# All visits in the small groups make the states' part of y on four tiles of TensorE, and VectorE adds the two parts; the first units' orders arranged anew

## The chip, the core and the metric

The kernel runs on one core of one Trainium2 chip. The metric is the device time of one execution in microseconds (us), the median of several runs. The profiled execution is one further run under the hardware profiler.

## The reference

A gated linear attention over (batch 4, 8 heads, 768 steps, head size 48) feeds two MLPs over 3072 tokens of width 384.

```
f = 1 / (1 + exp(-f_logit))
for t in range(S):
    state = f[t][:, None] * state + outer(k[t], v[t])
    y[t]  = q[t] @ state
x  = y.transpose(0, 2, 1, 3).reshape(B * S, H * D)          # 3072 x 384
x2 = ((1 / (1 + exp(-(x @ w_gate)))) * (x @ w_val)) @ w_out # d_ff 1536
h  = x2 @ w_in                                              # d_ff 2048
out = (h * (1 / (1 + exp(-1.702 * h)))) @ w_out2
```

## The kernel before

**Attention in units.** A unit is a pair of heads over 256 steps; there are 48 of them. Its 256 steps fall into four chunks of 64. For each unit ScalarE makes the gates (`forget`), VectorE their running product and its reciprocal (`prepare`: a scan and a reciprocal), GpSimd multiplies q by the one and k by the other (`decay_q`, `decay_k`), ScalarE scales q by the product at the end of the chunk before (`prepare_q`, into `q_in`) and takes the chunk ends out (`take_end`).

**Visits.** TensorE works on the units in visits, each for up to three units at different stages: unit n is turned (k transposed, `turn_ps`, and the scores k by q), unit n-1 has its products k by v (from which VectorE makes the states, `new_states`, four in a row), and unit n-2 has its y made: masked scores times v, and the states times `q_in`. The products stand in the two banks of `att_ps` (in the first visits also of `out_ps`). After a visit VectorE masks the scores and makes the states; ScalarE copies y to `y_t` (`take_y`); DMAs move it to `x_raw`, the input of the first MLP. There are 53 visits, v = 0 to 52; the first eight stand before the MLP.

**The MLPs.** All products are made of three fp32r products (high by high, low by high, high by low), so every operand is split: ScalarE casts the high part, VectorE subtracts to get the low part (`x_lo`, `act_lo`, `w_lo`). The tokens go in groups: two small ones of 256, then groups of 512. A group of the first MLP has 12 blocks (`j`); a block has 18 products up (gate and value, into `up_ps`), perhaps a visit, and then the 9 products out of the block before. For each block ScalarE makes the sigmoid (`act_f`), VectorE multiplies (`act_f`), ScalarE casts `act_hi`, VectorE subtracts `act_lo`. Groups 0 and 1 are the small ones: visits 8 to 12 stand in blocks 1, 2, 4, 6, 8 of group 0, visits 13 to 20 in blocks 0, 1, 3, 4, 5, 7, 8, 9 of group 1. In group 0 the weights of the first MLP are loaded and split, too: ScalarE casts `w_hi`, VectorE makes `w_lo`. The first piece of weights is split by GpSimd in thirds (`split_w1`).

**Order.** Each engine's instructions are written out by hand, and each engine runs them in order; semaphores connect the engines.

**Two ways to make y.** Up to visit 20 (`v < APART`) the states' products are added in PSUM to the same columns as the scores' part: TensorE waits until its own earlier products are drained (`tiles_done`), then adds 6 or 8 products, and ScalarE copies y once, 128 x 256. In visits 8 to 20 VectorE waits for that copy before it reads the banks (`copied_first`); elsewhere ScalarE waits until VectorE has read scores and products (`wait_products_read`). From visit 21 on the states' part goes to columns of its own (`STATE_COL`), on four tiles of TensorE without the drain; ScalarE copies that part in four copies of 48 x 128, and VectorE then adds the scores' part out of PSUM (`add_y`). SyncE's move of y and TensorE's next visit wait for `y_copied` in the one form and for `y_added` in the other (`wait_y`).

## Time and profile before

| | |
|---|---|
| median of 3 runs | 951.71 us (951.61 to 951.87) |
| profiled execution | 953.08 us, its span 951.0 us |
| TensorE matmul, busy | 934.9 us (98% of the span) |
| VectorE, busy | 487.0 us (51%) |
| ScalarE, busy | 375.3 us (39%) |
| GpSimd, busy | 105.8 us (11%) |
| chain that ended last | TensorE 95%, VectorE 2%, the rest below 2% each |

The span is the time from the first to the last instruction, and about 2 us of the execution lie around it. TensorE's share is that of the whole; in the first 31 us, where the first units are prepared, it is lower. A time in a timeline is counted from the start of the span. The first product of the MLP starts at 30.75 us; the third group's first visit starts at 141.7 us.

### The profile page before, as it was taken

Reading aid. Unit: us, or ns where it says so; the run is one execution under the profiler, and the core shown is the slowest. Engines: PE = TensorE matmul, PEld = TensorE weight load, DVE = VectorE, ACT = ScalarE, POOL = GpSimd, SP = SyncE. Lnnn points to the kernel's source line nnn. Section 1 sums busy time; section 2 is a strip of 40 time slices with the busy share of each in tenths; the row PEclk is TensorE's granted clock in tenths of the full one; section 3 lists DMA queues with packets and bytes.
Section 4 is the critical chain, followed back from the end, with each engine's and each line's share of the span. In section 5 each row is a group of like instructions: output and inputs, shape, how many; then the busy total and the mean of one; then the engine's idle time right before and its main releaser. Section 6 shows DMA issues by size and latency. Waiting matters only on the chain.

```text
span 951.0 us, 18139 instructions
## 1 busy us (share of the span) xinstructions
PE 934.9 (98%) x7203; PEld 781.2 (82%) x7203; DVE 487.0 (51%) x829; ACT 375.3 (39%) x941; POOL 105.8 (11%) x125
## 2 busy tenths in 40 slices
PE   7899999999999999999999999999999999999997
PEld 5899988888888888888888888888888888888885
DVE  7897776647665665664333234343443443433433
ACT  4665444543444444443424333233232333232332
POOL 4211211101110111110004420000000000000000
PEclk9899999999999999999999999999999999999999
DMA  5762322211112212120123320020010200100000
GB/s 146 201 188 60 85 64 61 64 47 58 57 48 54 80 52 51 29 80 21 63 69 98 99 84 1 1 67 1 24 43 1 68 1 1 66 1 1 34 1 35
DMA packets 44008, 52.36 MB, mean 55 GB/s; under 512 B 8464, under 2 KB 33808, under 8 KB 43920
## 3 DMA queue, kind: packets, MB, share of 16 engines
q1 hardware_dynamic: 41184, 43.30, 15.8%
q10 hardware_dynamic: 2736, 7.85, 2.9%
q8 instruction: 59, 0.97, 0.4%
q14 instruction: 29, 0.24, 0.1%
HBM read 36.96 MB, written 9.44 MB: 49 GB/s over the span
## 4 chain that ended last, share of the span: by engine, by line
PE 95%; DVE 2%; issue 1%; ACT 1%; DMA 1%; SPq 0%; ACTq 0%; POOL 0%; DVEq 0%; POOLq 0%
PE up_ps L1087 17%; PE up_ps L1088 17%; PE up_ps L1089 17%; PE out_ps L1087 13%; PE out_ps L1088 12%; PE out_ps L1089 12%; PE att_ps L1035 2%; PE att_ps L1057 1%; PE att_ps L1047 1%; PE turn_ps L1014 1%; PE up_ps L1003 1%; PE att_ps L1069 1%; PE att_ps L1080 1%; DMA x_raw<-y_t 1%; DVE inv_prod L811 1%
## 5 line engine op out<-in xcount | busy, mean ns | idle before, releaser
L1087 PE MATMUL up_ps<-x_hi,w_hi 128*128 128x512 f32 (+1 forms) x792 | 293.7, 371 | 1.5 <-DVE x_lo L867 0.8
L1089 PE MATMUL up_ps<-x_hi,w_lo 128*128 128x512 f32 (+1 forms) x792 | 293.2, 370 | 0.0
L1088 PE MATMUL up_ps<-x_lo,w_hi 128*128 128x512 f32 (+1 forms) x792 | 293.1, 370 | 0.0
L1087 PE MATMUL out_ps<-act_hi,w_hi 128*128 128x512 f32 (+1 forms) x540 | 208.0, 385 | 0.8 <-DVE act_lo L932 0.8
L1088 PE MATMUL out_ps<-act_lo,w_hi 128*128 128x512 f32 (+1 forms) x540 | 203.2, 376 | 0.0
L1089 PE MATMUL out_ps<-act_hi,w_lo 128*128 128x512 f32 (+1 forms) x540 | 202.9, 376 | 0.0
L718 ACT CAST act_hi<-act_f 128x512 fp32r<-128x512 f32 (+1 forms) x180 | 106.6, 592 | 232.1 <-DVE act_f L923 159.7
L932 DVE TENSOR_TENSOR act_lo<-act_f,act_hi 128x512 fp32r<-128x512 f32 (+1 forms) x180 | 118.1, 656 | 113.8 <-ACT act_hi L718 113.8
L1087 PEld LDWEIGHTS up_ps<-x_hi,w_hi 128*128 128x128 f32 x792 | 149.7, 189 | 27.8 <-DVE x_lo L867 1.3
L1089 PEld LDWEIGHTS up_ps<-x_hi,w_lo 128*128 128x128 f32 x792 | 149.6, 189 | 25.3
L1088 PEld LDWEIGHTS up_ps<-x_lo,w_hi 128*128 128x128 f32 x792 | 149.7, 189 | 25.0
L926 DVE TENSOR_TENSOR act_f<-act_f,up_ps 128x512 f32<-128x512 f32 x96 | 66.0, 688 | 173.3 <-ACT act_f L714 173.3
L714 ACT ACTIVATE act_f<-up_ps 128x512 f32<-128x512 f32 x96 | 57.4, 598 | 192.9 <-PE up_ps L1089 192.9
L1087 PEld LDWEIGHTS out_ps<-act_hi,w_hi 128*128 128x128 f32 x540 | 101.8, 188 | 22.2 <-DVE act_lo L932 1.2
L1089 PEld LDWEIGHTS out_ps<-act_hi,w_lo 128*128 128x128 f32 x540 | 102.0, 189 | 18.6
L1088 PEld LDWEIGHTS out_ps<-act_lo,w_hi 128*128 128x128 f32 x540 | 102.0, 189 | 16.9
L923 DVE TENSOR_TENSOR act_f<-act_f,up_ps 128x512 f32<-128x512 f32 (+1 forms) x84 | 50.3, 599 | 112.5 <-PE up_ps L1089 103.9
L811 DVE RECIPROCAL inv_prod<-prod 128x256 f32<-128x256 f32 x48 | 84.1, 1752 | 1.6
L712 ACT ACTIVATE act_f<-up_ps 128x512 f32<-128x512 f32 (+1 forms) x84 | 45.1, 537 | 62.7 <-PE up_ps L1089 60.7
L506 POOL TENSOR_TENSOR q_dec<-q_raw,prod 128x256 f32<-128x256 f32 x48 | 35.3, 735 | 299.6 <-DVE prod L804 229.9
L639 ACT COPY y_t<-att_ps 48x128 f32<-48x128 f32 x128 | 33.3, 260 | 60.3 <-DVE state L840 59.2
L624 ACT ACTIVATE q_in<-q_dec,p_end 128x64 f32<-128x64 f32 x176 | 47.4, 339 | 0.9
(77 smaller groups left out, 577.7 us busy)
## 6 DMA issues: line engine op xcount, KB each, us to landing
stage<-w SPq DMA_DIRECT2D x16, 384.0 KB, 3.3
stage<-w ACTq DMA_DIRECT2D x9, 576.0 KB, 4.3
q_raw<-q_t SPq DMA_DIRECT2D x96, 48.0 KB, 1.9
k_raw<-k_t SPq DMA_DIRECT2D x96, 48.0 KB, 1.9
v_raw<-v_n SPq DMA_DIRECT2D x48, 96.0 KB, 2.2
x_raw<-x_dram SPq DMA_DIRECT2D x6, 768.0 KB, 5.0
out_t<-final SPq DMA_DIRECT2D x18, 256.0 KB, 2.1
f_raw<-f_t SPq DMA_DIRECT2D x82, 48.0 KB, 1.9
```

What stands on the lines that cost most here:

```text
L506: pool.tensor_tensor(q_dec[:, n % 4, :], q_raw[:, u.s, :], prod[:, u.s, :], ALU.mult).then_inc(q_dec_done, 1)
L624: last = act.mul(q_in[:, n % 2, at], q_dec[:, n % 4, at], end_before(u, c))
L712: act.activation(act_f[:, b.t, 0:b.n], up_ps[:, 0, 0:b.n], ACT.Sigmoid).then_inc(sig_done, 1)
L714: act.activation(act_f[:, b.t, 0:b.n], up_ps[:, b.j % 2, 0:b.n], ACT.Sigmoid, scale=1.702).then_inc(sig_done, 1)
L718: act.copy(act_hi[:, b.t, 0:b.n], act_f[:, b.t, 0:b.n]).then_inc(act_hi_done, 1)
L811: dve.reciprocal(inv_prod[:, u.s, :], prod[:, u.s, :]).then_inc(inv_done, 1)
L923: dve.tensor_tensor(act_f[:, b.t, 0:b.n], act_f[:, b.t, 0:b.n], up_ps[:, 1, 0:b.n], ALU.mult).then_inc(mul_done, 1)
L926: dve.tensor_tensor(act_f[:, b.t, 0:b.n], act_f[:, b.t, 0:b.n], up_ps[:, b.j % 2, 0:b.n], ALU.mult).then_inc(mul_done, 1)
L932: dve.tensor_tensor(act_lo[:, b.t, 0:b.n], act_f[:, b.t, 0:b.n], act_hi[:, b.t, 0:b.n].bitcast(F32), ALU.subtract).then_inc(act_split, 1)
L1087: pe.matmul(dst, w_hi[:, at:at + P], m_hi, start=first, stop=False)
L1088: pe.matmul(dst, w_hi[:, at:at + P], m_lo, start=False, stop=False)
L1089: return pe.matmul(dst, w_lo[:, at:at + P], m_hi, start=False, stop=last)
```

## The change

It has four parts.

1. Every visit from the eighth on (that is, all visits in the small groups too) makes the states' part of y in columns of its own; ScalarE copies that part in four copies and VectorE adds the scores' part. Only the visits before the MLP keep the old form. This concerns visits 9 to 20, twelve in number (visit 8 makes no y). Where the unit is the first of its sequence, two products with a state of zeros are added.
2. In all visits ScalarE copies first, as soon as the visit is done, and VectorE waits for the copy before it reads the banks.
3. On ScalarE and VectorE the first units' steps are in another order: `forget` of units 2 to 5 and the loads of f and w1 come earlier, `prepare(2)` comes ahead of the first visit's mask.
4. On GpSimd a third of the first weights is split before `decay_k(3)`, and two waits for the states are gone.

```diff
-
-    APART = VISIT_AT[2, 0]
...
-        def wait_products_read(eng, v):
-
-            turned, kept, _ = VISITS[v]
-            if turned is not None:
-                eng.wait_ge(scores_masked, turned + 1)
-            if kept is not None:
-                eng.wait_ge(state_done, CH * (kept + 1))
-
-        def copied_first(v):
-
-            return BEFORE_MLP <= v < APART
-
         def wait_y(eng, n):
 
-            if out_visit[n] < APART:
+            if out_visit[n] < BEFORE_MLP:
                 eng.wait_ge(y_copied, n + 1)
             else:
-                eng.wait_ge(y_added, len([m for m in range(n + 1) if out_visit[m] >= APART]))
+                eng.wait_ge(y_added, n - UG + 1)
...
-                    pool.wait_ge(w1_hi_done, 1)
+                    if part == 0:
+                        pool.wait_ge(w1_hi_done, 1)
                     pool.tensor_tensor(w_lo[:, at], w1_staged(0)[:, at], w_hi[:, at].bitcast(F32),
                                        ALU.subtract).then_inc(w1_thirds, 1)
 
...
                 decay(0)
                 decay(1)
                 decay(2)
-                decay(3)
-
-                pool.wait_ge(state_done, CH * 2)
+                decay_q(3)
                 split_w1(0)
+                decay_k(3)
                 split_w1(1)
                 decay_q(4)
-                pool.wait_ge(state_done, CH * 4)
                 split_w1(2)
                 decay_k(4)
                 decay(5)
...
                 def take_y(n):
                     v = out_visit[n]
                     act.wait_ge(visit_done, v + 1)
-                    if not copied_first(v):
-                        wait_products_read(act, v)
                     wait(act, y_moved[n % YS], 16 * moves(n % YS, n))
                     y = y_t[:, n % YS, :].rearrange("p (c r t) -> p c r t", c=BLOCKS, r=SIDES)
-                    if v < APART:
+                    if v < BEFORE_MLP:
                         act.copy(y, banks(v)[:, :, Y_COL:STATE_COL].rearrange("p r (c t) -> p c r t", c=BLOCKS)).then_inc(y_copied, 1)
                         return
                     for i in range(PAIR):
...
                 first_load_f(2)
                 forget(1)
                 first_load_f(3)
+                forget(2)
                 take_end(0)
                 take_k(0)
-                forget(2)
+                forget(3)
                 first_load_f(4)
+                load_w1(0)
+                prepare_q(0)
                 take_end(1)
-                prepare_q(0)
                 take_k(1)
-                forget(3)
-                load_w1(0)
+                first_load_f(5)
+                take_end(2)
+                forget(4)
                 prepare_q(1)
-                take_end(2)
                 take_k(2)
-                first_load_f(5)
+                load_w1(1)
                 w1_first_part(0)
                 take_y(0)
                 take_end(3)
+                prepare_q(2)
                 take_k(3)
-                load_w1(1)
-                prepare_q(2)
-                forget(4)
+                forget(5)
                 take_y(1)
                 prepare_q(3)
                 first_load_f(6)
                 load_w1(2)
-                forget(5)
                 take_y(2)
                 first_move_y(2, slice(2, None))
                 take_y(3)
...
                 def add_y(n, v):
 
 
-                    dve.wait_ge(y_copied, n + 1)
                     y = y_t[:, n % YS, :].rearrange("p (c r t) -> p r c t", c=BLOCKS, r=SIDES)
                     dve.tensor_tensor(y, y, banks(v)[:, :, Y_COL:STATE_COL].rearrange("p r (c t) -> p r c t", c=BLOCKS),
                                       ALU.add).then_inc(y_added, 1)
...
                 def after_visit(v):
                     turned, kept, made = VISITS[v]
                     dve.wait_ge(visit_done, v + 1)
-                    if made is not None and copied_first(v):
-                        wait_y(dve, made)
+                    if made is not None:
+                        dve.wait_ge(y_copied, made + 1)
                     if turned is not None:
                         mask(turned, v)
                     if kept is not None:
                         new_states(kept, v)
-                    if made is not None and v >= APART:
+                    if made is not None and v >= BEFORE_MLP:
                         add_y(made, v)
...
                 dve.wait_ge(gaps_set, 8)
                 prepare(0)
                 prepare(1)
+                prepare(2)
                 after_visit(0)
-                prepare(2)
                 after_visit(1)
                 prepare(3)
                 after_visit(2)
...
-                    if made is not None and v < APART:
+                    if made is not None and v < BEFORE_MLP:
 
                         last.then_inc(tiles_done, 1)
                         pe.wait_ge(tiles_done, made + 1)
```

A visit on TensorE in block 4 of the first small group, before (`scores` times `v_raw` and `q_in` by `state` make y):

```order
L1035 MATMUL att_ps<-scores,v_raw 48x64 [waits y_copied,scores_masked,state_done]
L1035 MATMUL att_ps<-scores,v_raw 48x64 x7
L1047 MATMUL att_ps<-v_raw,k_rows 64x48 [waits v_loaded2,k_rows_done]
L1047 MATMUL att_ps<-v_raw,k_rows 64x48 x7
L1057 MATMUL att_ps<-q_dec,k_dec 64x64 [waits q_dec_done]
L1057 MATMUL att_ps<-q_dec,k_dec 64x64 x7
L1069 MATMUL att_ps<-q_in,state 48x64 [waits q_in_done,state_done,tiles_done]
L1069 MATMUL att_ps<-q_in,state 48x64 x7
```

The same visit after the change:

```order
L1017 MATMUL att_ps<-scores,v_raw 48x64 [waits y_added,scores_masked,state_done]
L1017 MATMUL att_ps<-scores,v_raw 48x64 x7
L1029 MATMUL att_ps<-v_raw,k_rows 64x48 [waits v_loaded2,k_rows_done]
L1029 MATMUL att_ps<-v_raw,k_rows 64x48 x7
L1039 MATMUL att_ps<-q_dec,k_dec 64x64 [waits q_dec_done]
L1039 MATMUL att_ps<-q_dec,k_dec 64x64 x7
L1062 MATMUL att_ps<-q_in,state 48x64 [waits q_in_done,state_done]
L1062 MATMUL att_ps<-q_in,state 48x64 x7
```

The wait for `tiles_done` is gone, and the wait at the visit's first product into `att_ps` is for `y_added`, not for `y_copied`.

ScalarE around the same visit, from `act_hi` of block 4 to the next sigmoid, before:

```order
L718 CAST act_hi<-act_f 128x256 [waits act_used,mul_done]
L607 COPY k_rows<-turn_ps 128x256 [waits k_turned]
L612 COPY p_end<-prod 128x4 [waits scan_done]
L635 COPY y_t<-att_ps 128x256 [waits y_moved2,visit_done]
L624 ACTIVATE q_in<-q_dec,p_end 128x64 [waits p_end_done,visit_done,q_dec_done]
L624 ACTIVATE q_in<-q_dec,p_end 128x64 x3
L588 ACTIVATE gate<-f_raw 128x4x63 [waits scan_done,f_loaded0]
L589 ACTIVATE floor<-f_raw 128x4
L569 CAST w_hi<-final 128x1152 [waits w1_loaded3]
L563 DMA stage<-w 128x1152 [waits w1_split]
```

And after:

```order
L701 CAST act_hi<-act_f 128x256 [waits act_used,mul_done]
L592 COPY k_rows<-turn_ps 128x256 [waits k_turned]
L597 COPY p_end<-prod 128x4 [waits scan_done]
L622 COPY y_t<-att_ps 48x2x64 [waits y_moved2,visit_done]
L622 COPY y_t<-att_ps 48x2x64 x3
L609 ACTIVATE q_in<-q_dec,p_end 128x64 [waits p_end_done,visit_done,q_dec_done]
L609 ACTIVATE q_in<-q_dec,p_end 128x64 x3
L573 ACTIVATE gate<-f_raw 128x4x63 [waits scan_done,f_loaded0]
L574 ACTIVATE floor<-f_raw 128x4
L554 CAST w_hi<-final 128x1152 [waits w1_loaded3]
L548 DMA stage<-w 128x1152 [waits w1_split]
```

One copy of y has become four, and they stand in the same place, ahead of `q_in`, the gates of a later unit, a weight's high part and the sigmoid (`act_f`).

VectorE behind the mask of that visit, before:

```order
L822 TENSOR_TENSOR scores<-att_ps,causal 128x256 [waits y_copied,visit_done]
L840 SCALAR_TENSOR_TENSOR state<-state,p_end,att_ps 128x48 [waits p_end_done]
L840 SCALAR_TENSOR_TENSOR state<-state,p_end,att_ps 128x48 [waits state_done] x3
L923 TENSOR_TENSOR act_f<-act_f,up_ps 128x256 [waits value_ready,sig_done]
L874 TENSOR_TENSOR w_lo<-final,w_hi 128x1152 [waits w1_hi_done]
L932 TENSOR_TENSOR act_lo<-act_f,act_hi 128x256 [waits act_hi_done]
```

And after:

```order
L805 TENSOR_TENSOR scores<-att_ps,causal 128x256 [waits y_copied,visit_done]
L823 SCALAR_TENSOR_TENSOR state<-state,p_end,att_ps 128x48 [waits p_end_done]
L823 SCALAR_TENSOR_TENSOR state<-state,p_end,att_ps 128x48 [waits state_done] x3
L830 TENSOR_TENSOR y_t<-y_t,att_ps 128x2x2x64
L905 TENSOR_TENSOR act_f<-act_f,up_ps 128x256 [waits value_ready,sig_done]
L856 TENSOR_TENSOR w_lo<-final,w_hi 128x1152 [waits w1_hi_done]
L914 TENSOR_TENSOR act_lo<-act_f,act_hi 128x256 [waits act_hi_done]
```

The add of y stands behind the states and ahead of the next block's `act_f`.

GpSimd in the front, from `q_dec` of unit 3 to `k_dec` of unit 4, before:

```order
L506 TENSOR_TENSOR q_dec<-q_raw,prod 128x256 [waits scan_done,q_loaded1]
L514 TENSOR_TENSOR k_dec<-k_raw,inv_prod 128x256 [waits visit_done,inv_done,k_loaded1]
L526 TENSOR_TENSOR w_lo<-stage,w_hi 128x384 [waits w1_hi_done,state_done]
L526 TENSOR_TENSOR w_lo<-stage,w_hi 128x384 [waits w1_hi_done]
L506 TENSOR_TENSOR q_dec<-q_raw,prod 128x256 [waits visit_done,scan_done,q_loaded0]
L526 TENSOR_TENSOR w_lo<-stage,w_hi 128x384 [waits w1_hi_done,state_done]
L514 TENSOR_TENSOR k_dec<-k_raw,inv_prod 128x256 [waits visit_done,inv_done,k_loaded0]
```

And after:

```order
L492 TENSOR_TENSOR q_dec<-q_raw,prod 128x256 [waits scan_done,q_loaded1]
L513 TENSOR_TENSOR w_lo<-stage,w_hi 128x384 [waits w1_hi_done]
L500 TENSOR_TENSOR k_dec<-k_raw,inv_prod 128x256 [waits visit_done,inv_done,k_loaded1]
L513 TENSOR_TENSOR w_lo<-stage,w_hi 128x384
L492 TENSOR_TENSOR q_dec<-q_raw,prod 128x256 [waits visit_done,scan_done,q_loaded0]
L513 TENSOR_TENSOR w_lo<-stage,w_hi 128x384
L500 TENSOR_TENSOR k_dec<-k_raw,inv_prod 128x256 [waits visit_done,inv_done,k_loaded0]
```

The first third of `w_lo` has moved ahead of `k_dec` of unit 3, and no third waits for `state_done` any more.

## Rows read from the trace of the kernel before

**Rows 1.** Busy time by stretch: us, then each engine, granted clock, DMA share, GB/s.

```profile
31.00:80.00 49.00, 45.95 (x593) 43.75 (x593) 45.75 (x72) 30.16 (x85) 9.05 (x13) 0.97 0.57 163
80.00:141.00 61.00, 60.00 (x874) 55.78 (x873) 43.10 (x92) 28.85 (x102) 11.38 (x16) 1.00 0.27 72
141.00:450.00 309.00, 309.00 (x3150) 254.09 (x3149) 189.70 (x341) 138.97 (x434) 43.15 (x58) 1.00 0.20 54
```

**Rows 2.** Timeline of TensorE, a small group's visit (start us, length us, what).

```profile
53.48 0.43 PE L1057 MATMUL att_ps<-q_dec,k_dec 48*64 48x64 f32 x16
...
54.58 0.39 PE L1087 MATMUL out_ps<-act_hi,w_hi 128*128 128x256 f32 x1
```

**Rows 3.** Timeline of TensorE, a large group's visit.

```profile
142.47 0.43 PE L1057 MATMUL att_ps<-q_dec,k_dec 48*64 48x64 f32 x16
...
143.05 0.39 PE L1087 MATMUL out_ps<-act_hi,w_hi 128*128 128x256 f32 x1
```

**Rows 4.** Timeline of ScalarE, blocks 6 and 7 of the first small group.

```profile
62.93 0.41 ACT L718 CAST act_hi<-act_f 128x256 fp32r<-128x256 f32 x1 [2.27 <-DVE act_f L923]
...
63.61 0.38 ACT L635 COPY y_t<-att_ps 128x256 f32<-128x256 f32 x1
...
66.28 0.39 ACT L712 ACTIVATE act_f<-up_ps 128x256 f32<-128x256 f32 x1
```

**Rows 5.** Timeline of VectorE, first small group (in brackets: idle before, releaser).

```profile
49.72 0.42 DVE L923 TENSOR_TENSOR act_f<-act_f,up_ps 128x256 f32<-128x256 f32 x1 [0.55 <-PE up_ps L1089]
...
62.54 0.36 DVE L923 TENSOR_TENSOR act_f<-act_f,up_ps 128x256 f32<-128x256 f32 x1
...
64.95 0.41 DVE L822 TENSOR_TENSOR scores<-att_ps,causal 128x256 f32<-128x256 f32 x1
...
66.70 0.42 DVE L923 TENSOR_TENSOR act_f<-act_f,up_ps 128x256 f32<-128x256 f32 x1 [0.26 <-ACT act_f L712]
```

**Rows 6.** Timeline of ScalarE, the four copies of y in a large group.

```profile
145.77 1.08 ACT L639 COPY y_t<-att_ps 48x128 f32<-48x128 f32 x4 [1.92 <-DVE state L840]
```

**Rows 7.** Timeline of VectorE, the add in a large group.

```profile
146.88 0.42 DVE L848 TENSOR_TENSOR y_t<-y_t,att_ps 128x256 f32<-128x256 f32 x1 [1.27 <-ACT y_t L639]
```

**Rows 8.** Waits of VectorE, 80 to 140 us: us in total, times, longest.

```profile
DVE scores L822 <- ACT y_t L635: 3.8, 8, 0.9
```

**Rows 9.** Timeline of VectorE, second small group.

```profile
93.39 0.42 DVE L822 TENSOR_TENSOR scores<-att_ps,causal 128x256 f32<-128x256 f32 x1 [0.29 <-ACT y_t L635]
...
95.30 0.42 DVE L923 TENSOR_TENSOR act_f<-act_f,up_ps 128x256 f32<-128x256 f32 x1 [0.41 <-PE up_ps L1089]
...
114.10 0.42 DVE L923 TENSOR_TENSOR act_f<-act_f,up_ps 128x256 f32<-128x256 f32 x1 [1.28 <-PE up_ps L1089]
...
127.57 0.42 DVE L923 TENSOR_TENSOR act_f<-act_f,up_ps 128x256 f32<-128x256 f32 x1 [1.40 <-PE up_ps L1089]
...
132.68 0.42 DVE L923 TENSOR_TENSOR act_f<-act_f,up_ps 128x256 f32<-128x256 f32 x1 [1.52 <-PE up_ps L1089]
```

**Rows 10.** Timeline of SyncE's DMA issues, the last visit before the third group.

```profile
131.92 1.16 SPq L401 DMA_DIRECT2D x_raw<-y_t  x2
```

**Rows 11.** Timeline of VectorE, front.

```profile
20.21 0.69 DVE L804 TENSOR_TENSOR_SCAN prod<-gate,floor 128x256 f32<-128x256 f32 x1 [2.00 <-ACT floor L589]
```

**Rows 12.** Timeline of ScalarE, front.

```profile
16.18 1.15 ACT L569 CAST w_hi<-stage 128x1152 fp32r<-128x1152 f32 x1 [1.19 <-DMA stage<-w]
```

**Rows 13.** Timeline of GpSimd, front.

```profile
17.05 0.72 POOL L514 TENSOR_TENSOR k_dec<-k_raw,inv_prod 128x256 f32<-128x256 f32 x1 [1.05 <-issue]
18.28 1.96 POOL L526 TENSOR_TENSOR w_lo<-stage,w_hi 128x384 fp32r<-128x384 f32 x2 [0.51 <-DVE state L840]
```

**Rows 14.** Chain that ended last, front: start us, length us, what.

```profile
26.52 4.93 DMA x_raw<-y_t
```

**Rows 15.** Timeline of TensorE, the first visit that makes y in a small group.

```profile
43.06 0.44 PE L1035 MATMUL att_ps<-scores,v_raw 64*48 64x64 f32 x16 [1.49 <-issue]
```

**Rows 16.** Busy time by stretch, behind that visit.

```profile
44.00:49.00 5.00, 4.95 (x40) 4.88 (x41) 4.89 (x9) 3.34 (x11) 1.15 (x2) 0.66 0.26 45
```

## The prediction

> **What bounds the kernel now.** I read the share of each engine by stage first, then the timelines of the engines that wait on each other there. From 141 us on TensorE is busy for all of the time [rows 1], so nothing that the edit does to the large groups' visits can come out there, unless it makes TensorE wait. What can move the end lies before 141 us: the front, up to the first MLP product at about 31 us, and the two small groups (256 tokens; blocks of 27 products), 31 to 141 us. There VectorE is nearly as full as TensorE: 45.75 against 45.95 us of the 49 us up to 80 us, 43.10 against 60.00 us in the 61 us behind them [rows 1]. The first small group (weights are split in it too) is thus bound by two things at once, the second mostly by TensorE with stretches that VectorE holds up.
>
> **The visits on TensorE.** In a small group's visit the next out product starts 1.10 us behind the start of the scores' products (53.48 to 54.58) [rows 2]; in a visit of the large groups, whose form the small ones now take, 0.58 us behind it (142.47 to 143.05) [rows 3]. The drain wait and the two-bank form go: 0.52 us for each of the 12 visits (v = 9 to 20), 6.2 us in all. For the three units of a batch's first step two more matmuls of 64 columns are added, some hundredths each. This is a gain only where TensorE is what the others wait for.
>
> **What the same visits cost ScalarE and VectorE.** ScalarE's one copy of y (0.38 us) [rows 4] becomes four, which take 1.08 us in the large groups [rows 6]: 0.70 us more. VectorE adds the states' part afterwards: 0.42 us, of which some 0.34 us are its own when the next operation starts overlapped [rows 7].
>
> In the first small group ScalarE works without a gap from act_hi at 62.93 over the copy of y at 63.61 to the next sigmoid at 66.28 [rows 4], and VectorE's next act_f waits 0.26 us for that sigmoid [rows 5]. So ScalarE's 0.70 us are on the path from act_f at 62.54 to act_f at 66.70. VectorE's add is hidden: it fits in the 0.26 us and the 0.70 us of new idle. Its mask at 64.95 isn't delayed, as the four copies would end at 63.61 + 1.08 = 64.69. Behind it VectorE is back to back, so nothing is given back, and TensorE, 0.52 us quicker, waits for the sigmoid. Three visits are like this (blocks 4, 6, 8): 2.1 us. At block 2 VectorE waited 0.55 us for TensorE before 49.72 [rows 5], part of which covers the longer chain: I count 0.4 of the 0.7 us. The first visit makes no y. The sum for the first small group is +2.5 us. It is at least +2.0 (TensorE, relieved, catches up some of it at the end of the group) and at most +3.3 us, if an operation behind the copies doesn't overlap with them and each visit costs 0.1 us more, and block 2 the whole.
>
> In the second small group VectorE waits for the copy of y at all eight visits, 3.8 us in total [rows 8]. Where the copy stands right behind ScalarE's other work, that wait is 0.29 us, as at 93.39 [rows 9], and the four copies move the mask by some 0.66 us. Where the wait is longer (3.8 - 8 x 0.29 = 1.5 us in all), the copy had waited for the visit's end, which now comes 0.52 us sooner, and that much is covered. So the masks come 8 x 0.66 - 1.5 = 3.8 us later and the adds bring 8 x 0.34 = 2.7 us: 6.5 us on VectorE's chain. Four of the visits have idle behind them in which VectorE waited for TensorE, 0.41, 1.28, 1.40 and 1.52 us [rows 9], and the earlier TensorE lets the chain use it up: 0.4 + 1.3 + 1.4, and 1.0 at the last, where TensorE's own saving is the floor. That takes 4.1 us off, which leaves 2.4; rounded, +2.5 us. The other four are followed by the scan and the reciprocal of the next unit and then act_f, all back to back, and pass their 0.5 to 1.0 us on. Bounds: +1.0 us if TensorE gets ahead in all of it, +4.0 us if the next visit, which may only start once the add is done (its wait changes from y_copied to y_added), stretches the cycle as well.
>
> The moves of y to x_raw wait for the add instead of the copy, and behind them in SP's queue are v, q and k. At the last visit before the third group VectorE was free at 132.68 - 1.52 = 131.16 and would now be at 131.7, while SP only issued that move at 131.92 [rows 10], late for its own queue: I count nothing. Without that cover it would cost up to 0.5 us, inside the bound above.
>
> A rule to weigh: the Trainium skill ("ScalarE: Activation LUTs", section "What ACT_TABLE_LOAD costs") gives an ACTIVATE with immediate scale 186 ns + 0.833 ns per element, 93 ns of it overlapped when back to back. By that four of 128 elements would take about 0.49 us more than one of 256 and the small groups would come to some +2.5 us in place of +5.0. The case has the same copies at 1.08 us, so the row decides.
>
> **The large groups.** ScalarE now copies before the mask, where it used to wait for VectorE's states, and VectorE no longer waits 1.27 us for the four copies [rows 7]. Both gain, neither is waited for: TensorE is busy throughout [rows 1]. Nothing. It could be below nothing only if TensorE had stalls there, and it has none.
>
> **The front.** VectorE waited 2.00 us for the gate of unit 4 before the scan at 20.21 [rows 11], and ScalarE's second copy of y waited for VectorE's mask and states. Both go: forget(4) stands ahead of take_y(0), and take_y no longer waits for mask and states. Against it, GpSimd now splits a third of w1 ahead of k_dec of unit 3. That third needs w_hi, made from 16.18 for 1.15 us [rows 12], and takes about 1 us, after which k_dec takes 0.7; k_dec started at 17.05 before, the splits at 18.28 [rows 13]. With the old w_hi, k_dec would start at 18.3; the load of w1 is issued about 1 us sooner, which leaves 0 to 1.2 us of delay for visit 3. What ends the front is the last piece of x: it was issued at 26.52, behind the fourth y, and landed 4.93 us later [rows 14]. The fourth y hangs on the states of unit 3, which follow visit 3 on VectorE with its idle taken out. I take -0.5 us, from -2.0 (all of VectorE's idle comes through) to +0.8 us (visit 3 late, nothing else).
>
> **TensorE's clock.** Between 44 and 49 us the granted clock is 0.66, a mean of both levels, 1.2 and 2.4 GHz [rows 16], behind a wait of 1.49 us at 43.06 [rows 15]. With TensorE waiting 1 to 2 us at several visits of the small groups I expect the lower level more often. As TensorE then has time to spare, most of it is hidden: +0.5 us, from 0 to +2.5.
>
> **Sum.** -0.5 + 2.5 + 2.5 + 0 + 0.5 = +5.0 us. The profiled execution took 953.08 us (span 951.0 and about 2 around it) and would become 958.1; the median of the runs is 951.71, 1.4 us below it, so I forecast **956.7 us**. Its own range is 953.5 to 960.5.
>
> **The rivals.**
> *TensorE's saving counts.* If the other engines had room, 12 x 0.52 = 6.2 us would go and the front's 0.5 us with it: 945.0 us. For it: TensorE is 98% busy in the second small group, and its visits get shorter for certain. Against it: the idle times on VectorE are too small [rows 5, 8]. It decides if less than some 0.3 us per visit of the copies' 0.70 us and the add reach the path. The Trainium skill ("TensorEngine Tiling (Array Packing)", "Performance Considerations") says that tiling quickens TensorE and not the emptying of PSUM, which may become the bottleneck. By the promise of up to 2x the sum would be this rival's, by the warning it is the forecast; the rows on ScalarE bear out the warning. Chance 0.10, with lesser gains of the same kind.
> *The front pays for it.* The front gains 2.0 us or more, TensorE catches up in both small groups (+2.0 and +1.0), and the clock stays: +1.0 us, 952.7 us, which can't be told from no change. For it: 2.00 us of idle are taken out [rows 11]. Against it: visit 3 is held by GpSimd, and the last DMA by its own landing. Chance 0.15.
> *The wait for y_added and the clock make it worse.* The next visit waits for the add in the pairs of neighbouring visits, TensorE stands for 1 to 2 us each time and falls to 1.2 GHz behind it: +0.5 + 3.3 + 4.0 + 2.5, about +10 us, 962 us. Chance 0.12; the forecast itself has 0.63.
>
> A measurement of this kernel tells a change from none at about 0.2%, 1.9 us. From the cases: faster 0.10, within 0.2% 0.14, slower 0.76. The range of 8 in 10 leaves out the gain and the far end of the last rival: 952.0 to 961.5 us.
>
> **What would show it.** Right: in the first small group the distance from act_f of blocks 4, 6 and 8 to the next act_f is 4.9 us in place of 4.16, with idle before it put down to ScalarE's sigmoid; TensorE shows idle before up products (releaser: the sigmoid) and, in the second small group, before the visits' first matmul (releaser: VectorE's y); the visit itself is 0.5 us shorter; from the third group on both timelines run alike at a fixed distance. Wrong: act_f of block 0 earlier by 2 us or more, TensorE without idle in 80 to 141 us, or 1.27 us of TensorE idle that appears in the large groups.

## The result, and the profile after

The changed kernel takes 960.2 us (median of 6 runs, 958.75 to 960.7) against 951.87 us (951.61 to 952.35): ratio 1.0084, 95% interval 1.0071 to 1.0097, slower by 8.3 us. Forecast were 956.7 us, +5.0. The profiled execution took 960.7 us, its span 958.7.

Where the time went is read from the starts of VectorE's first multiplication (act_f) in the blocks. Before: block 0 of the first small group at 34.60, of the second at 84.84, of the third group at 142.20. After: 35.58, 89.16 and 149.43. So the front costs +0.98 us in these two executions, the first small group +3.34, the second +2.91 (57.36 to 60.27). From there to VectorE's last copies the distance stays: 7.23 us at the third group, 7.26 at the end (944.63 before, 951.89 after).

Busy time by stretch, after, in the columns of [rows 1]:

```profile
31.00:80.00 49.00, 41.81 (x593) 39.59 (x594) 43.28 (x73) 33.32 (x97) 8.09 (x11) 1.00 0.55 162
80.00:141.00 61.00, 55.23 (x882) 52.40 (x881) 43.50 (x97) 32.76 (x121) 10.30 (x14) 1.00 0.26 71
141.00:450.00 309.00, 308.42 (x3099) 254.01 (x3098) 194.14 (x346) 137.19 (x438) 45.08 (x60) 1.00 0.20 56
```

TensorE and VectorE are both less busy up to 80 us, and from 80 to 141 us TensorE is idle for 5.8 of 61 us where it was idle for 1.0. What TensorE waits for, over the whole span:

```profile
engine line waited for: us in total, times, longest us
PE up_ps L1069 <- ACT act_f L695: 7.3, 7, 1.3
PE att_ps L1017 <- DVE y_t L830: 4.2, 4, 1.5
PE turn_ps L996 <- DVE state L823: 3.9, 1, 3.9
```

The first row is ScalarE's sigmoid, late in both small groups; the second is VectorE's add, ahead of four visits of the second group; the third stands in the front, and its releaser is named wrongly (below). The visit itself is 0.52 us shorter, as foreseen: from the start of the products k by q to the next product out 0.58 us, against 1.10 in [rows 2]. TensorE in a block of the first small group, after:

```profile
73.26 0.43 PE L1039 MATMUL att_ps<-q_dec,k_dec 48*64 48x64 f32 x16
73.51 0.40 PE L1062 MATMUL att_ps<-q_in,state 48*48 48x64 f32 x16
73.84 0.38 PE L1069 MATMUL out_ps<-act_hi,w_hi 128*128 128x256 f32 x1
```

ScalarE in such a block, to be laid beside [rows 4]:

```profile
65.42 0.41 ACT L701 CAST act_hi<-act_f 128x256 fp32r<-128x256 f32 x1 [2.53 <-DVE act_f L905]
65.73 0.37 ACT L592 COPY k_rows<-turn_ps 128x256 f32<-128x256 f32 x1
65.99 0.20 ACT L597 COPY p_end<-prod 128x4 f32<-128x4 f32 x1
66.09 1.07 ACT L622 COPY y_t<-att_ps 48x128 f32<-48x128 f32 x4
67.19 0.35 ACT L609 ACTIVATE q_in<-q_dec,p_end 128x64 f32<-128x64 f32 x1
...
68.56 1.14 ACT L554 CAST w_hi<-stage 128x1152 fp32r<-128x1152 f32 x1
69.72 0.38 ACT L695 ACTIVATE act_f<-up_ps 128x256 f32<-128x256 f32 x1
```

The queue is without a gap from act_hi to the sigmoid, and from the first copy to the next operation it is 1.10 us (66.09 to 67.19). Before, with one copy at 63.61 [rows 4], it is 0.26 us:

```profile
63.87 0.36 ACT L624 ACTIVATE q_in<-q_dec,p_end 128x64 f32<-128x64 f32 x1
```

VectorE in the same block, after:

```profile
65.02 0.36 DVE L905 TENSOR_TENSOR act_f<-act_f,up_ps 128x256 f32<-128x256 f32 x1
...
67.45 0.41 DVE L805 TENSOR_TENSOR scores<-att_ps,causal 128x256 f32<-128x256 f32 x1
67.78 1.15 DVE L823 SCALAR_TENSOR_TENSOR state<-state,p_end,att_ps 128x48 f32<-128x48 f32 x4
68.85 0.41 DVE L830 TENSOR_TENSOR y_t<-y_t,att_ps 128x256 f32<-128x256 f32 x1
70.13 0.42 DVE L905 TENSOR_TENSOR act_f<-act_f,up_ps 128x256 f32<-128x256 f32 x1 [0.88 <-ACT act_f L695]
```

From act_f to act_f it is 5.11 us in place of 4.16, and behind the add VectorE still stands for 0.88 us: the add is hidden there, the copies are not. In the second small group it is another picture. VectorE's waits, 80 to 140 us, to be laid beside [rows 8], and VectorE from one act_f to the next, over a visit (block 3):

```profile
DVE scores L805 <- ACT y_t L622: 8.3, 8, 1.3
```

```profile
104.39 0.36 DVE L905 TENSOR_TENSOR act_f<-act_f,up_ps 128x256 f32<-128x256 f32 x1
105.23 0.43 DVE L914 TENSOR_TENSOR act_lo<-act_f,act_hi 128x256 fp32r<-128x256 f32 x1 [0.47 <-ACT act_hi L701]
106.64 0.42 DVE L805 TENSOR_TENSOR scores<-att_ps,causal 128x256 f32<-128x256 f32 x1 [0.98 <-ACT y_t L622]
106.98 1.16 DVE L823 SCALAR_TENSOR_TENSOR state<-state,p_end,att_ps 128x48 f32<-128x48 f32 x4
108.05 0.41 DVE L830 TENSOR_TENSOR y_t<-y_t,att_ps 128x256 f32<-128x256 f32 x1
108.38 0.68 DVE L787 TENSOR_TENSOR_SCAN prod<-gate,floor 128x256 f32<-128x256 f32 x1
109.10 1.75 DVE L794 RECIPROCAL inv_prod<-prod 128x256 f32<-128x256 f32 x1
110.77 0.36 DVE L905 TENSOR_TENSOR act_f<-act_f,up_ps 128x256 f32<-128x256 f32 x1
```

Here VectorE itself closes the loop: its mask waits 0.98 us for the copies (3.8 us in all before, 8.3 now), and the mask, the states, the add, the scan and the reciprocal follow back to back up to the next act_f, on which ScalarE's next act_hi and copies hang.

The front. GpSimd and TensorE:

```profile
17.23 1.00 POOL L513 TENSOR_TENSOR w_lo<-stage,w_hi 128x384 fp32r<-128x384 f32 x1 [2.57 <-ACT w_hi L554]
18.18 0.73 POOL L500 TENSOR_TENSOR k_dec<-k_raw,inv_prod 128x256 f32<-128x256 f32 x1
```

```profile
18.96 0.69 PE L996 MATMUL turn_ps<-ident,k_dec 128*128 128x128 f32 x2 [3.87 <-DVE state L823]
```

The third of w1 waits for ScalarE's cast, and k_dec(3) waits behind it: it starts at 18.18 instead of 17.05 [rows 13], though its input, the reciprocal, is done at 15.57. TensorE's turn starts right behind the end of k_dec (18.91). The trace puts the wait down to VectorE's states, which end at the same moment; the runs below tell them apart. From 17 to 24 us the granted clock is 0.50, the lower level (1.2 GHz), and 1.00 before the change. It stays at the lower level from about 16.8 to 30.4 us; before the change from about 24.3 to 27.7 us. VectorE's mask of visit 3, which stood behind VectorE's 2.00 us of idle [rows 11] before, now waits for TensorE:

```profile
22.60 0.42 DVE L805 TENSOR_TENSOR scores<-out_ps,causal 128x256 f32<-128x256 f32 x1 [2.19 <-PE att_ps L1029]
```

### The profile page after: what moved, and what is told of

The parts are those of the page before. It is cut to its first block, busy times and chain, and to the rows that moved or that the text cites. A ratio compares the mean times of both kernels' runs of the same rounds, so it can differ in the third digit from the quotient of the medians.

```text
span 958.7 us, 18217 instructions
## 1 busy us (share of the span) xinstructions
PE 932.8 (97%) x7219; PEld 779.6 (81%) x7219; DVE 491.5 (51%) x841; ACT 381.0 (40%) x977; POOL 105.7 (11%) x125
## 4 chain that ended last, share of the span: by engine, by line
PE 87%; DVE 4%; issue 4%; ACT 3%; DMA 1%; SPq 1%; POOL 0%; ACTq 0%; DVEq 0%; POOLq 0%
PE up_ps L1069 16%; PE up_ps L1071 16%; PE up_ps L1070 16%; PE out_ps L1069 12%; PE out_ps L1070 11%; PE out_ps L1071 11%; PE att_ps L1017 1%; PE up_ps L985 1%; PE att_ps L1039 1%; DVE act_f L905 1%; PE turn_ps L996 1%; DVE prod L787 1%; ACT y_t L622 1%; PE att_ps L1029 1%; PE att_ps L1062 1%
## 5 line engine op out<-in xcount | busy, mean ns | idle before, releaser
L823 DVE SCALAR_TENSOR_TENSOR state<-state,p_end,att_ps 128x48 f32<-128x48 f32 x170 | 44.7, 263 | 5.2 <-ACT y_t L622 0.3
```

What stands on the lines that cost most here:

```text
L823: dve.scalar_tensor_tensor(out=after[:, c, :], in0=state_before(u, c), scalar=end_before(u, c), in1=products, op0=ALU.mult, op1=ALU.add).t ...
```

## The experiments

All times are medians. "First" is the distance between the act_f of block 0 of the first and of the second small group, "second" that from there to the third group's, both of the profiled execution; among kernels with the same edits in the groups they repeat to 0.2 us (but for the first group before, see E5). The start of block 0 doesn't: among kernels with the same front it differs by 0.7 to 2.4 us (31.12 to 33.56 in E2, E7, E10, E11 and E12), and the 12 runs of E6 lie between 949.4 and 953.8 us. So what the front costs is read from the medians, which rest on 5 to 12 runs each; a difference of two of them is good to some 1 us, an estimate from the scatter of the runs. One number in the table is out of line: in the profiled execution of the kernel before, the first product of the MLP starts 3.85 us ahead of block 0's act_f (30.75 to 34.60), with a wait for x_lo in between; after the change and in E1, E2, E3, E5, E6 and E7 it is 2.50 or 2.51 us. So block 0 before stands some 1.3 us late in that execution.

| | median, us | ratio to before, interval | block 0 at | first | second |
|---|---|---|---|---|---|
| before | 951.9 | | 34.60 | 50.24 | 57.36 |
| after | 960.2 | 1.0084 (1.0071 to 1.0097) | 35.58 | 53.58 | 60.27 |
| E1 | 958.0 | 1.0065 (1.0052 to 1.0079) | 33.49 | 53.47 | 60.33 |
| E2 | 957.4 | 1.0062 (1.0048 to 1.0076) | 31.12 | 53.61 | 60.29 |
| E3 | 960.3 | 1.0088 (1.0075 to 1.0102) | 35.99 | 53.60 | 60.27 |
| E4 | 949.6 | 0.9976 (0.9965 to 0.9988) | 35.01 | 49.70 | 54.49 |
| E5 | 951.3 | 0.9994 (0.9986 to 1.0003) | 32.62 | 49.63 | 57.36 |
| E6 | 952.6 | 1.0005 (0.9995 to 1.0015) | 34.87 | 49.76 | 57.33 |
| E7 | 951.1 | 0.9991 (0.9982 to 0.9999) | 33.40 | 49.77 | 57.36 |
| E8 | 957.8 | 1.0066 (1.0053 to 1.0079) | 34.93 | 53.59 | 58.86 |
| E9 | 956.7 | 1.0046 (1.0033 to 1.0060) | 34.87 | 50.68 | 60.17 |
| E10 | 954.9 | 1.0033 (1.0021 to 1.0045) | 33.19 | 50.68 | 60.29 |
| E11 | 951.7 | 0.9991 (0.9982 to 1.0000) | 33.56 | 49.19 | 57.36 |
| E12 | 952.2 | 1.0000 (0.9991 to 1.0009) | 31.23 | 50.69 | 57.01 |

**E1, the new visits with the old orders.**

```diff
 GpSimd:  -decay_q(3)  split_w1(0)  decay_k(3)
          +decay(3)    split_w1(0)          # and both waits for the states
 ScalarE, VectorE: the front's lists as before the change
```

> The changed kernel with the kernel before's orders at the front on ScalarE, GpSimd and VectorE: only the visits are changed. My theory: the change's time is made of three parts, read at the starts of VectorE's first multiplications: the front +1.0 us, the first small group +3.3, the second +2.9. With the old front this kernel should stand 6 to 7 us above the kernel before (958.2 to 958.9 us), and its block 0 should start within 0.3 us of 34.6. Rival A (the front is a mere shift that the small groups take back, since they wait for other things): it comes out like the changed kernel, 960.2. Rival B (the new orders at the front are needed to feed the new visits): over 961.

The time was 958.0 us, and the groups are those of the changed kernel. The visits alone make 6.1 of the 8.3 us; the new orders at the front make the other 2.2 (960.2 less 958.0). Block 0 stood at 33.49, 1.1 us ahead of the expected 34.6, which the late block 0 of the kernel before accounts for; E5 tests another theory.

**E2, k_dec(3) first.**

```diff
 decay_q(3)
+decay_k(3)
 split_w1(0)
-decay_k(3)
```

> The changed kernel with one line moved: on GpSimd unit 3's k_dec ahead of the first third of w1's low part. My theory: TensorE's wait of 3.87 us ahead of the turn of k_dec(3) at 18.96 is the wait for that k_dec, which stands behind the split from 17.23 although its input is there from 15.57. The wait should shrink to 1 to 2 us, VectorE's first multiplication of block 0 should come 1 to 2.5 us earlier than 35.58, and the time should be 958.0 to 959.3. Rival (the front is bounded by ScalarE's w1 part and x_hi, which stand behind): block 0 stays within 0.3 us and the time at 960.2.

2.8 us came back, more than expected. GpSimd and TensorE in E2:

```profile
15.74 0.72 POOL L500 TENSOR_TENSOR k_dec<-k_raw,inv_prod 128x256 f32<-128x256 f32 x1
```

```profile
16.52 0.44 PE L996 MATMUL turn_ps<-ident,k_dec 128*128 128x128 f32 x2 [1.44 <-DVE state L821]
```

The turn follows k_dec's start by 0.78 us here, in the changed kernel and in the kernel before alike, so it hangs on k_dec and not on the states that the trace names. E2's profiled execution was the fastest of its five (956.0 against the median of 957.4), so its block 0 at 31.12 is not typical.

**E3, TensorE kept busy.**

```diff
-keep_warm({0: 2, 1: 5, 2: 2, 4: 2, 6: 8, 7: 8}.get(v, 0))
+keep_warm({0: 2, 1: 5, 2: 30, 4: 2, 6: 8, 7: 8}.get(v, 0))
```

> The changed kernel with 30 identity products of padding instead of 2 behind visit 2, so that TensorE is busy in most of the 3.87 us in which it waits for k_dec(3). Theory 1 (the clock): TensorE's long idleness there is followed by 13.65 us at the lower of its two clock levels, which costs the front about 1 us: with the padding the lower stretch goes or shrinks, block 0 starts 0.7 to 1.5 us earlier than 35.58, and the time is 958.7 to 959.5. Theory 2 (the wait itself): block 0 starts within 0.3 us of 35.58 or later, whatever the clock does, and the time stays at 960.2 or above.

The time stayed, but the experiment overshot. TensorE in E3:

```profile
14.78 6.96 PE L981 MATMUL up_ps<-ident 128*128 128x128 f32 x60
21.59 0.38 PE L996 MATMUL turn_ps<-ident,k_dec 128*128 128x128 f32 x2
```

The padding lasted 6.96 us, so visit 3 came 2.63 us later than in the changed kernel, at the full clock, and block 0 only 0.41 us later. So 2.2 us came back. TensorE's waits between that turn and the MLP tell from what; first the changed kernel's only one, then E3's:

```profile
24.14 0.68 PE L1017 MATMUL out_ps<-scores,v_raw 64*48 64x64 f32 x16 [0.51 <-issue]
```

```profile
25.49 0.44 PE L1017 MATMUL out_ps<-scores,v_raw 64*48 64x64 f32 x16 [1.20 <-issue]
```

From the turn to the first product of the MLP it is 14.12 us in the changed kernel (18.96 to 33.08) and 11.89 us in E3 (21.59 to 33.48), with the same instructions. The changed kernel had only 0.51 us of idle there, and E3 had more, so a later visit's slack can't have given the 2.2 us back: the clock did. In the changed kernel all of this stretch up to 30.4 us runs at the lower level, in E3 some 3 to 4 us of it. In these two executions the lower level thus costs the front 2.2 us.

**E4, one copy of four.**

```diff
-for i in range(PAIR):
-    for r in range(SIDES):
+for i in range(1):          # in the small groups
+    for r in range(1):
```

> The changed kernel with only one of ScalarE's four copies of the states' part of y in each visit of the small groups (the other three quarters of y's states' part are left out there). TensorE's tiles and VectorE's add stay. My theory: the small groups pay because ScalarE's next sigmoid stands behind four copies (1.10 us to the next instruction) instead of one (0.26): with one copy the first group's blocks 4, 6 and 8 should come at 4.16 to 4.2 us after their predecessors in place of 5.11, the group should lose 0.4 to 0.9 us in place of 3.3, the second group 1 to 2 in place of 2.9, and the time should be 955 to 957. Rival (VectorE's add of 0.53 us sets the group, or TensorE's visit on four tiles): the first group still loses over 2.5 us and the time stays over 959.

The largest effect of all: 949.6 us, 10.6 us below the changed kernel and below the kernel before, too, in a kernel that leaves three quarters of the states' part of y out. Block 4 and its like came at 4.16 us again. ScalarE in E4:

```profile
63.59 0.26 ACT L622 COPY y_t<-att_ps 48x128 f32<-48x128 f32 x1
63.80 0.35 ACT L609 ACTIVATE q_in<-q_dec,p_end 128x64 f32<-128x64 f32 x1
...
65.17 1.14 ACT L554 CAST w_hi<-stage 128x1152 fp32r<-128x1152 f32 x1
66.22 0.37 ACT L695 ACTIVATE act_f<-up_ps 128x256 f32<-128x256 f32 x1
```

Three copies less are 3.9 us in the first small group and 5.8 in the second; the other 0.9 us lie outside the groups. What is left of the change there (the short visit, and the add) is worth 2.9 us in the second group (54.49 against 57.36) and nothing in the first (49.70 against 49.63 in E5). The expectation had the second group still losing.

**E5, the old kernel copying y first in the front too.**

```diff
 def copied_first(v):
-    return BEFORE_MLP <= v < APART
+    return v < APART
```

> The kernel before with one condition changed: in the visits ahead of the MLP too, ScalarE copies y ahead of VectorE's mask and states instead of behind them. E1, with the old orders, had block 0 at 33.49 against 34.60 before. Theory: that gain is the copy that no longer waits for VectorE (here the only edit): block 0 at 33.3 to 33.8, the groups' intervals as before, time 950.5 to 951.1. Rival: the 1.1 us of E1 come from elsewhere (a profiled execution that was luckier with its DMAs), and block 0 stays at 34.4 to 34.8 and the time at 951.8.

951.3 us, interval up to 1.0003: not told from the kernel before. Block 0 stood 2 us earlier in the one profiled execution, 1.3 us of which are the late x of the kernel before; the median moved by 0.7 us, and the first group is 0.6 us shorter in the traces (49.63 against 50.24). There block 2 takes 4.16 us where it took 4.45 before, and the granted clock from 44 to 49 us is 1.00 instead of 0.66 [rows 16]. The wait ahead of it was 1.81 us here and 1.49 us before, so the longer of the two waits was not followed by the lower level.

**E6, the new front with the old visits.** E5, and the changed kernel's lists for the front on ScalarE, GpSimd and VectorE.

> The kernel before with the changed kernel's orders at the front on ScalarE, GpSimd and VectorE and with y copied first there; its visits in the groups are the old ones. Theory: the new orders cost the front 2.1 us (35.58 in the changed kernel against 33.49 in E1) and copying first gives 1.1 back, so block 0 is at 35.3 to 35.8, the small groups go as before, and the time is 952.4 to 953.2. Rival (the front's loss needs the new visits): block 0 under 34.6 and the time at or under 951.8.

952.6 us, inside the expected range but not told from the kernel before (interval 0.9995 to 1.0015), and 1.4 above E5. Block 0, at 34.87, was ahead of the expected 35.3. With E1 there are two pairs that differ in the orders and GpSimd's two waits alone: +2.2 and +1.4 us (+2.0 and +1.1 by the means of the same runs).

The traces of E5 and E6 show where it goes. TensorE's turn of unit 3 starts at 17.77 and 17.81 us, so k_dec(3) was not late in E6, whose load of w1 landed early (cast at 14.85 us). But the first product of the MLP starts at 30.11 and at 32.37 us, 2.26 us later, and the granted clock from 17 to 24 us is 1.00 in E5 and 0.50 in E6.

**E7, E6 with k_dec(3) first.** The same edit as E2.

> E6 with unit 3's k_dec ahead of the first third of w1's low part on GpSimd, as in E2: the kernel before with the changed kernel's front, less its late k_dec, and without its visits. Theory (the parts add up): block 0 at 31.1 as in E2, 3.5 us earlier than before, the groups as before, time 948.0 to 949.0, faster than both kernels. Rival (an early front meets w1's loads, which then come late in the first group): the first group's intervals grow and over 1 us of the 3.5 is given back, time over 949.4.

951.1 us, 1.6 below E6, and faster than the kernel before by 0.09% (0.9982 to 0.9999): the best complete kernel here, by a hair. The expectation, 948 to 949, took E2's block 0 at 31.12 for typical; it was a lucky execution. In E7 k_dec(3) waited 0.86 us for the load of k and started at 16.38 us, not at 15.74. Repaired, the new front isn't worth more than the old one (951.1 against E5's 951.3).

**E8, a small add.**

```diff
+if v < VISIT_AT[2, 0]:
+    y, scored = y[:, :, :, 0:1], scored[:, :, :, 0:1]
 dve.tensor_tensor(y, y, scored, ALU.add)
```

> The changed kernel with VectorE's add in the small groups cut to one column of each block of 64 tokens (the other columns of the states' part of y are left unadded there). ScalarE keeps its four copies. My theory after E4: both small groups are bounded by ScalarE's copies, so an add that is shorter gives 0 in the first group and 0 to 0.7 us in the second, time 959.4 to 960.2. Rival (the second group's step as predicted: 2.7 of the added time is VectorE's adds): the second group regains 2 to 3 us and the time is 957.2 to 958.3.

The first group didn't move (53.59), the second gave back 1.41 us, between the two expectations; the time lies in the rival's range (957.2 to 958.3). VectorE's add in E8, block 0:

```profile
92.35 0.15 DVE L833 TENSOR_TENSOR y_t<-y_t,att_ps 128x4 f32<-128x4 f32 x1
```

The add is 0.26 us shorter, and each of the blocks 0, 3, 4 and 7 is shorter by just that (7.54 to 7.28, 6.38 to 6.12, 6.31 to 6.05, 6.31 to 6.05). In these four blocks of the second group VectorE's add is on the path in full; block 9 gained 0.31 us, and the blocks 1, 5 and 8 gained 0.1 us or less. The median fell by 2.4 us; the last 1.0 us of that lies outside the groups, within the front's scatter.

**E9, ScalarE's other work moved ahead of act_hi.**

```diff
 act.activation(act_f, up_ps, ACT.Sigmoid)
+if visited:                  # from block 4 of the first group on
+    w1_first_part(b.j + AHEAD); forget(FORGET_AT[b.g, b.j])
 act.wait_ge(mul_done, q + 1)
 act.copy(act_hi, act_f)
```

> The changed kernel with two of ScalarE's jobs moved in the blocks with a visit (from block 4 of the first group on): w1's high part (1.05 to 1.16 us) and the gates of a later unit (0.5 to 0.6) stand between the block's sigmoid and its act_hi, where ScalarE is idle 2.5 us, and not behind the four copies. Nothing is left out. Theory (after E4 and E8 ScalarE's queue behind the copies is what lengthens the groups): the first group's 5.12 us intervals fall to 4.16 to 4.4, the second group loses up to 4 us against the changed kernel's 60.27, time 953.5 to 956. Rival (the blocks wait for the copies themselves, by VectorE's mask behind y_t): the intervals stay over 4.8 and the time over 958.

ScalarE in E9:

```profile
61.11 1.14 ACT L554 CAST w_hi<-stage 128x1152 fp32r<-128x1152 f32 x1
62.15 0.41 ACT L573 ACTIVATE gate<-f_raw 128x252 f32<-128x252 f32 x1
62.47 0.20 ACT L574 ACTIVATE floor<-f_raw 128x4 f32<-128x4 f32 x1
63.74 0.41 ACT L708 CAST act_hi<-act_f 128x256 fp32r<-128x256 f32 x1 [1.07 <-DVE act_f L912]
...
66.60 0.38 ACT L695 ACTIVATE act_f<-up_ps 128x256 f32<-128x256 f32 x1
```

The blocks 4, 6 and 8 are back at 4.16 us with all four copies in place, and the group gave back 2.90 us. So it was ScalarE's queue behind act_hi, not the copies as such. The second group stayed at 60.17: there the copies hold VectorE's mask (8.4 us in all), and moving the gates from behind them gives nothing. The time, 956.7, is just outside the expected 953.5 to 956, since the second group was expected to gain.

**E10, both repairs.** E9 with E2's edit.

> E9 with unit 3's k_dec first on GpSimd as in E2: the whole change with both of its costs treated. Theory (the parts add): E9's time less 2.0 to 2.8 us, 951 to 953.5. Rival (ScalarE's new order in the groups already gives back what the front gains): within 1 us of E9.

1.8 us below E9, just short of the expected 2.0, and like E9 above the time expected (954.9 against 951 to 953.5). With E2 and E7 that makes three pairs for k_dec(3): 2.8, 1.6 and 1.8 us (2.5, 1.4 and 1.3 by the means).

**E11, the same two jobs moved in the old visits.** E7 with E9's edit.

> E7 (the old visits, the changed front with k_dec(3) first) with the same two jobs of ScalarE moved ahead of act_hi in the blocks with a visit. Theory: the old visits too wait for ScalarE (TensorE's wait for the sigmoid in each of the first group's 4.16 us blocks), but the 0.3 us of idle TensorE that E4 left there is all there is to get: the first group gains 0.3 us in each of 3 blocks, the second 0 to 3, time 948 to 950.5, the fastest of all. Rival: TensorE and VectorE bound the old visits, time within 0.5 us of 951.1.

The first group gained 0.58 us (49.19 against 49.77), less than the expected 0.9, the second nothing; 951.7 us, above the expected 948 to 950.5 and no better than E7 (0.6 us above it, where the rival said within 0.5). The rival is right for the second group.

**E12, the copies ahead of act_hi.** E10, and in the second small group:

```diff
+if b.g == 1:
+    take_y(made)            # the gates back in their place
 act.wait_ge(mul_done, q + 1)
 act.copy(act_hi, act_f)
```

> E10 with one further move, in the second small group alone: ScalarE's four copies of y stand ahead of the block's act_hi instead of behind it and k_rows, into ScalarE's idle time there (0.9 to 1.5 us before act_hi), and its gates stand where the changed kernel has them. Nothing is left out. Theory: the second group is set by the loop act_hi, k_rows, p_end, four copies on ScalarE, then mask, states, add, scan and reciprocal on VectorE, then act_f. With the copies done by act_hi VectorE's mask waits 0 to 0.3 us instead of 0.98 and more in each of 8 blocks, blocks 3 and 4 fall from 6.3 us to 5.3 to 5.6, the group from 60.3 to 54 to 57, and the time from 954.9 to 949 to 952. Rival (copying at once holds ScalarE till the visit ends, and act_hi, act_lo and TensorE's products behind them come late): the group stays over 58.5 and the time over 953.3.

The group fell from 60.29 to 57.01 us, block 4 from 6.32 to 5.25. VectorE in E12:

```profile
103.95 0.43 DVE L924 TENSOR_TENSOR act_lo<-act_f,act_hi 128x256 fp32r<-128x256 f32 x1 [0.47 <-ACT act_hi L711]
104.29 0.42 DVE L815 TENSOR_TENSOR scores<-att_ps,causal 128x256 f32<-128x256 f32 x1
```

The mask follows act_lo at once. Block 0, though, went from 7.54 to 8.24 us, and block 3 only from 6.38 to 6.16. ScalarE in block 0 of the second group:

```profile
83.16 1.07 ACT L622 COPY y_t<-att_ps 48x128 f32<-48x128 f32 x4 [2.01 <-PE att_ps L1072]
84.25 0.41 ACT L711 CAST act_hi<-act_f 128x256 fp32r<-128x256 f32 x1
```

It waits 2.01 us for the visit's end ahead of the copies, and act_hi starts 2.33 us behind block 0's act_f (81.92), where it was 0.46 us in E10. That is the rival's mechanism, in some blocks. The time is 952.2 us, just above the expected 949 to 952: the change's visits with their costs treated are not told from the kernel before (0.9991 to 1.0009), and don't beat it.

Not tried: letting VectorE mask while ScalarE copies. The two would read the same PSUM banks with nothing to order them.

## Why the prediction was right, and where it was wrong

**First small group, +2.5 forecast, +3.34 measured.** Mechanism right: the four copies lengthen ScalarE's queue up to the sigmoid (E4, E9), and the add is hidden (E8: 0). The mis-sized term is the 0.70 us per visit: it was the difference of two busy times, 1.08 and 0.38 us, while what counts is the distance to the next operation, 1.10 against 0.26, and the sigmoid behind the cast starts 1.16 us behind that cast's start where it was 1.05 in E4. Each visit cost 0.96 us, at the upper bound of 3.3 us that was given for exactly that. Block 2 paid 0.67 us in place of the 0.4 foreseen; in E5, at the full clock, its old form took 0.29 us less, so that against that its price was 0.96 us, too.

**Second small group, +2.5 forecast, +2.91 measured.** The chain was named rightly: masks later, adds in the chain, the scan and reciprocal pass them on. Its terms were 3.8 us for later masks, 2.7 for the adds, 4.1 absorbed. The masks' waits grew by 4.5 us (3.8 to 8.3). E8 took 0.26 us out of each add's 0.34 and got 1.41 back, so the eight adds carry about 1.41 x 0.34 / 0.26 = 1.8 us of the path, an estimate. Of the four waits for TensorE [rows 9], 4.6 us in all, one of 0.48 us is left after the change, so 4.1 us were used up, as foreseen. The masks' term was 0.7 us too small and the adds' term some 0.9 too large; part of the agreement is luck.

One count was wrong without consequence: by the kernel four units of the small groups (12 to 15), not three, are the first of their sequence and get the two added products.

**The two rules that were weighed.** By the Trainium skill ("ScalarE: Activation LUTs", section "What ACT_TABLE_LOAD costs") the four copies would cost some 0.49 us more than one, an estimate; the measured distances say 0.84. The Trainium skill's warning that the emptying of PSUM may become the bottleneck when TensorE is tiled ("TensorEngine Tiling (Array Packing)", section "Performance Considerations") is borne out: E4 shows 10.6 us between four copies and one, 9.7 of them in the small groups.

**TensorE's saving.** The rival of 945.0 us lost, but not because the saving is worth nothing: with ScalarE's three extra copies gone it is 2.9 us net of the adds in the second group (E4). It was paid for twice over by the copies.

**The front, -0.5 forecast: the step that failed.** It weighed VectorE's 2.00 us of idle [rows 11] as a gain, took visit 3's delay as 0 to 1.2 us, and named the landing of x's last piece as the end of the front. The delay came out at 1.13 us, near the end given, in the profiled execution. The gain didn't come: E5, E6 and E7 show that copying first and the earlier gates bring nothing that a median shows, and the mask behind that idle now waits 2.19 us for TensorE. And the front ended with TensorE's own queue: from the turn of unit 3 to the first product of the MLP TensorE idles for 0.51 us only, and its products and padding there run at the lower clock level. In the profiled executions that cost 2.2 us (E3), and E6 lost 2.26 us against E5 behind a turn that was on time. The prediction's front had no term for the clock.

k_dec(3) behind the split costs 1.6 to 2.8 us (E2, E7, E10). Its position ties visit 3 to the landing of w1's load: in the traces of E2, E7 and E10 the turn came 2.44, 0.65 and 0.91 us earlier, and the stretch from the turn to the MLP was 2.0, 0.8 and 0.8 us shorter. The whole front costs 1.4 to 2.2 us by medians. The bound of +0.8 us was too small.

**The clock, +0.5 forecast.** In the small groups the granted clock is 1.00 throughout, in spite of TensorE's waits of up to 1.80 us; before the change it had cost 0.29 us at block 2. The term belonged in the front, where it was 2.2 us in the profiled execution. Why the clock falls there earlier than before the change stays open: it falls behind the waits of 3.87 and 2.77 us (after, E6), but also behind a turn that had waited 1.13 us in E1, and not there in E5, whose wait is 1.13 us, too.

**Large groups, 0 forecast, 0 measured** (7.23 us at their start, 7.26 at their end).

The sum was 3.3 us too low, and the measured time lies near the upper end of the range: by the medians some 2.5 us are missing in the front, 0.8 and 0.4 in the groups, less the 0.5 that was put down for the clock. The forecast of a loss of this size rests on the two groups, whose mechanisms were right. The signs told beforehand were all seen: 5.11 us between act_f (4.9 foreseen), idle of VectorE and TensorE put down to the sigmoid, and TensorE's waits for the add.

## What to carry to other kernels

A faster form on a 98% busy engine pays only if its new helpers don't lengthen the queue of the engine that releases it: price an added instruction as the time to the next one's start on its engine, and ask which engine's queue runs without a gap between two steps of the loop. Where a queue is the bound, moving other work of the same engine into its idle time ahead of the loop's step can give the cost back without removing anything (E9: 2.90 of 3.34 us in the first group, nothing in the second, where it was the copies that held the next step). On the path, an instruction that waits for a load should not stand ahead of one that is ready (E2). And padding that keeps an engine busy stands in its queue like any work: at the lower clock level 16 identity products took 3.63 us here, at the full one 2.05.

## What the runs showed of the hardware

- A copy of 48 x 128 out of PSUM costs ScalarE 0.21 to 0.27 us to the next start, one of 128 x 256 0.26 us: between these two sizes the price goes by the number of instructions. Four small ones take 1.10 us.
- TensorE's turn of unit 3 lasted 0.44 us behind waits of 1.44 and 2.11 us (E2, E7) and 0.69 us, at the lower clock, behind 2.77 and 3.87 us (E6, after).
- A wait's length alone doesn't tell the clock behind it: at the first visit that makes y in a small group a wait of 1.49 us was followed by 0.66 granted (before), waits of 1.80 and 1.81 us by 1.00 (after, E1, E5, E6).
- The same TensorE instructions, from the turn of unit 3 to the MLP, took 14.12 us nearly all at the lower level and 11.89 us mostly at the full one (after, E3).
